# Whole-tile magnitudes taken in turn by ScalarE and VectorE, and the side work moved, in a long-convolution and MLP kernel

## The reference

```python
# part 1, per batch (2) over 12480 positions and 128 channels
h_filt = (np.maximum(pos_emb @ w1, 0.0) @ w2) * window
y = irfft(rfft(x * v, n=2*S) * rfft(h_filt, n=2*S))[:, :S]
x = (x * y).reshape(24960, 128)
# part 2
h = x @ w_in                      # 24960 x 2048
P = a[0] + a[1]*h + a[2]*h*h + a[3]*h*h*h
Q = 1.0 + abs(b[0])*abs(h) + abs(b[1])*h*h
out = (P / (Q + 1e-06)) @ w_out   # 24960 x 128
```

## Time and profile before

| what | value |
|---|---|
| median of 3 runs | 2174.0 us (2173.65 to 2177.25) |
| the profiled execution | 2174.0 us |
| its span in the trace | 2172.2 us |
| granted TensorE clock, mean | 0.983 |
| MLP stage, first slope to last slope | 630.1 to 2157.6 us |
| busy over the span | PE 92%, POOL 87%, DVE 84%, ACT 84% |

### The profile page before, as it was taken

One profiled execution on the slowest core, in us unless ns is written; L12 is line 12 of the kernel. 1 busy time (PEld: TensorE's weight loads), 2 busy tenths in 40 slices (PEclk: granted clock), 3 DMA queues, 4 the chain that ended last, 5 costly groups with the idle time before them and its releaser, 6 DMA issues. The chain is left out here.

```text
span 2172.2 us, 33906 instructions
## 1 busy us (share of the span) xinstructions
PE 2009.2 (92%) x8964; PEld 1463.6 (67%) x8964; DVE 1832.5 (84%) x2511; ACT 1824.1 (84%) x2671; POOL 1892.2 (87%) x1218
## 2 busy tenths in 40 slices
PE   7999499999959999999999999999999999999997
PEld 4777499999936666666666666666666666666664
DVE  4888488888849898989898988989888988898987
ACT  4888466666649998999999989999998989998998
POOL 3777398888839999999999999999999999999997
PEclk9999799999969999999999999999999999999999
DMA  6999766677531111111111111111111111111100
GB/s 178 312 305 309 191 162 172 178 181 180 128 86 31 31 31 31 30 31 30 31 30 31 34 31 31 30 33 50 36 31 31 30 31 30 31 30 31 30 13 12
DMA packets 65791, 175.60 MB, mean 81 GB/s; under 512 B 5046, under 2 KB 8414, under 8 KB 62686
## 3 DMA queue, kind: packets, MB, share of 16 engines
q1 hardware_dynamic: 65694, 174.67, 29.5%
HBM read 102.89 MB, written 71.76 MB: 80 GB/s over the span
## 5 line engine op out<-in xcount | busy, mean ns | idle before, releaser
L635 POOL TENSOR_TENSOR den<-slope,mag 128x832 f32<-128x832 f32 x480 | 948.1, 1975 | 43.4 <-POOL slope L627 4.6
L879 PE MATMUL acc_p<-g_s,w_out_k 128*128 128x416 f32 x1920 | 775.8, 527 | 61.3 <-DVE oT L801 38.5
L760 DVE SCALAR_TENSOR_TENSOR num<-square,level,h_p 128x832 f32<-128x832 f32 x480 | 517.7, 1078 | 116.2 <-ACT square L668 82.6
L627 POOL TENSOR_SCALAR slope<-mag,den_c 128x832 f32<-128x832 f32 x480 | 500.3, 1042 | 79.6 <-ACT mag L660 46.3
L879 PEld LDWEIGHTS acc_p<-g_s,w_out_k 128*128 128x128 f32 x1920 | 343.4, 190 | 315.5 <-issue 184.6
L793 DVE SCALAR_TENSOR_TENSOR g_s<-num,ratio,r_p 128x832 f32<-128x832 f32 x480 | 517.6, 1078 | 41.0 <-ACT r_p L684 26.8
L668 ACT ACTIVATE square<-h_p,centre 128x832 f32<-128x832 f32 x480 | 477.9, 996 | 7.7 <-DVE mag L755 5.3
L868 PE MATMUL h_p<-xy_hi,w_lo 128*128 128x416 f32 x960 | 448.5, 467 | 32.1 <-DVE num L760 29.5
L677 ACT ACTIVATE den<-den 128x832 f32<-128x832 f32 x480 | 450.1, 938 | 21.2 <-POOL den L635 21.1
L684 ACT ACTIVATE r_p<-den 128x832 f32<-128x832 f32 x480 | 436.2, 909 | 0.7 <-DVE g_s L793 0.7
L868 PE MATMUL h_p<-xy_lo,w_hi 128*128 128x416 f32 x960 | 338.0, 352 | 0.0
(11 more groups left out here) (79 smaller groups left out, 2807.9 us busy)
## 6 DMA issues: line engine op xcount, KB each, us to landing
bent<-bent_s SPq DMA_DIRECT2D x60, 576.0 KB, 6.2
bin_s<-bent SPq DMA_DIRECT2D x24, 1440.0 KB, 9.7
x_s<-in_x SPq DMA_DIRECT2D x60, 416.0 KB
back<-back_s SPq DMA_DIRECT2D x24, 960.0 KB, 7.8
vin_s<-back SPq DMA_DIRECT2D x30, 768.0 KB, 5.9
v_s<-in_v SPq DMA_DIRECT2D x30, 416.0 KB
out<-o_s SPq DMA_DIRECT2D x60, 208.0 KB
pos_s<-in_pos_emb SPq DMA_DIRECT2D x30, 88.0 KB
```

The costliest lines, as they stand in the source:

```text
L627: nc.gpsimd.tensor_scalar(slope[:, q % DEEP], mag[:, q % DEEP], den_c[:, 1:2], den_c[:, 0:1], ALU.mult, ALU.add).then_inc(slope_done, 1)
L635: nc.gpsimd.tensor_tensor(den[:, q % DEEP], slope[:, q % DEEP], mag[:, q % DEEP], ALU.mult).then_inc(den_done, 1)
L760: nc.vector.scalar_tensor_tensor(out=num[:, q % NUMS], in0=square[:, q % SQUARES], scalar=level[:], in1=h_p[:, q % 2, :, 0:TOK], op0=ALU.a ...
L879: mm = nc.tensor.matmul(acc_p[:, 0:TOK], w_out_k[:, ft], g_s[:, q % DEEP, t], start=(ft == 0), stop=(ft == FT - 1))
```

## The change

Four things are changed, all in the MLP stage:

- Whole tiles instead of halves: ACT takes the magnitude of even tiles (832 elements), DVE that of odd tiles. POOL waits for the one that made it. The square of an odd tile still waits for DVE's magnitude of this tile, the square of an even one no longer does.
- ACT's magnitude and square come right behind the reciprocal, ahead of leave and split_hi.
- DVE's sums stand at the head of a step, ahead of magnitude and activation; times_x and split_lo stand behind the numerator.
- PE's turn_in stands behind hidden and rows. The side work has other step numbers.

```diff
-            UNFOLD, TIMES_X, TURN_IN, SPLIT_HI, SPLIT_LO = (2, 5), (4, 7), (4, 7), (5, 8), (5, 8)
+            UNFOLD, TIMES_X, TURN_IN, SPLIT_HI, SPLIT_LO = (2, 6), (3, 7), (3, 7), (5, 9), (5, 9)
@@ pool, slopes
-                    pool.wait_ge(mag_act, G + 1)
-                    pool.wait_ge(mag_dve, G + 1)
+                    if q % 2:
+                        pool.wait_ge(mag_dve, i * (PER // 2) + q // 2 + 1)
+                    else:
+                        pool.wait_ge(mag_act, i * (PER // 2) + q // 2 + 1)
@@ act
-                    nc.scalar.activation(mag[:, q % DEEP, 0], h_p[:, q % 2, 0, 0:TOK], ACT.Abs).then_inc(mag_act, 1)
+                    nc.scalar.activation(mag[:, q % DEEP], h_p[:, q % 2, :, 0:TOK], ACT.Abs).then_inc(mag_act, 1)
 
                 def squared(i, q):
                     G = i * PER + q
                     act.wait_ge(h_done, G + 1)
-                    act.wait_ge(mag_dve, G + 1)
+                    if q % 2:
+                        act.wait_ge(mag_dve, i * (PER // 2) + q // 2 + 1)
...
                 def from_h(i, q):
-                    magnitude(i, q)
+                    if q % 2 == 0:
+                        magnitude(i, q)
                     squared(i, q)
@@ act, step
                     reciprocal(i, q)
+                    if ahead:
+                        from_h(i + (q + LEAD_E) // PER, (q + LEAD_E) % PER)
                     if m in LEAVE:
...
-                    if ahead:
-                        from_h(i + (q + LEAD_E) // PER, (q + LEAD_E) % PER)
@@ dve, magnitude
-                    nc.vector.tensor_scalar(mag[:, q % DEEP, 1].bitcast(I32), h_p[:, q % 2, 1, 0:TOK].bitcast(I32), NO_SIGN, None,
+                    nc.vector.tensor_scalar(mag[:, q % DEEP].bitcast(I32), h_p[:, q % 2, :, 0:TOK].bitcast(I32), NO_SIGN, None,
@@ dve, step
-                    if ahead:
-                        magnitude(i + (q + LEAD_E) // PER, (q + LEAD_E) % PER)
-                    activation(i, q)
                     if m in SUMS:
                         c = blk * BATCH + SUMS.index(m) - 1
                         if positive(c + 1):
                             sums(c)
-                    if more and m in TIMES_X:
-                        times_x(...)
-                    if more and m in SPLIT_LO:
-                        split_lo(...)
+                    if ahead and (q + LEAD_E) % 2:
+                        magnitude(i + (q + LEAD_E) // PER, (q + LEAD_E) % PER)
+                    activation(i, q)
                     if ahead:
                         numerator(i + (q + LEAD_E) // PER, (q + LEAD_E) % PER)
+                    side()          # times_x and split_lo, as above
@@ pe, step
                     project(i, q)
-                    if more and m in TURN_IN:
-                        turn_in(nxt + TURN_IN.index(m))
                     if ahead:
                         hidden(i + (q + LEAD_H) // PER, (q + LEAD_H) % PER)
                     if more and m in UNFOLD:
...
                         rows(nxt + half, i + (q // BLOCK_PAIRS + 1) // SLOTS, s, half, freed)
+                    if more and m in TURN_IN:
+                        turn_in(nxt + TURN_IN.index(m))
```

More of the change, by code:

```diff
@@ L808, in _ @@
                 for q in range(LEAD_E):
-                    magnitude(0, q)
+                    if q % 2:
+                        magnitude(0, q)
                     numerator(0, q)
@@ L813, in step @@
                     blk, m = i * SLOTS + q // BLOCK_PAIRS, q % BLOCK_PAIRS
-                    nxt, s = (blk + 1) * 2, (q // BLOCK_PAIRS + 1) % SLOTS
-                    if ahead:
-                        magnitude(i + (q + LEAD_E) // PER, (q + LEAD_E) % PER)
-                    activation(i, q)
                     if m in SUMS:
@@ L821, in step, with side @@
                             sums(c)
-                    if more and m in TIMES_X:
-                        times_x(nxt + TIMES_X.index(m), i + (q // BLOCK_PAIRS + 1) // SLOTS, s, TIMES_X.index(m))
-                    if more and m in SPLIT_LO:
-                        split_lo(nxt + SPLIT_LO.index(m), s, SPLIT_LO.index(m))
+                    if ahead and (q + LEAD_E) % 2:
+                        magnitude(i + (q + LEAD_E) // PER, (q + LEAD_E) % PER)
+                    activation(i, q)
+                    def side():
+                        nxt, s = (blk + 1) * 2, (q // BLOCK_PAIRS + 1) % SLOTS
+                        if more and m in TIMES_X:
+                            times_x(nxt + TIMES_X.index(m), i + (q // BLOCK_PAIRS + 1) // SLOTS, s, TIMES_X.index(m))
+                        if more and m in SPLIT_LO:
+                            split_lo(nxt + SPLIT_LO.index(m), s, SPLIT_LO.index(m))
                     if ahead:
                         numerator(i + (q + LEAD_E) // PER, (q + LEAD_E) % PER)
+                        side()
+                    else:
+                        side()
                 for q in range(PER):
```

## The result

The changed kernel takes 2199.1 us (median of 4 runs, 2197.7 to 2200.1), against 2174.5 for the kernel before on the same chip: ratio 1.011, 95% interval 1.0093 to 1.0128. It is slower, as forecast, but by 25 us and not by 94: only a quarter of the forecast loss came. The time lies 7 us above the low end of the range. The span of the profiled execution is 2195.5 us.

A forecast was written before the change was run, and what follows sets the result against it. A ring through ACT and DVE was to bound the MLP stage: 239.5 x 6.45 = 1544.8, + 23.8 splits + 22.4 loop gap + 30 sums = 1621.0 us against 1527.5. Forecast 2268 us, range 2192 to 2300.

The forecast's parts named there:

- The ring: MLP stage, ACT and DVE waiting in turn over an even and an odd tile: 6.45 us per two steps.
- split_hi: On ACT at steps 5 and 9, between odd square and logarithm: 0.41 us each, 58 times, 23.8 us.
- the sums at m = 8: On DVE ahead of activation, behind PE's late project: the numerator 1.0 us late, 30 times, 30 us.
- the leaves: On ACT at steps 2 and 14, behind the even square: 0.47 us each, hidden in a 0.75 us wait.
- DVE side work: times_x and split_lo behind an odd numerator on DVE, 0.6 us: hidden within 0.1 us.
- the wait for turn_in: ACT's wait for PE at split_hi: 1.53 x 4 = 6.1 us per 32 steps, forecast to go.
- Rival 1: MLP stage: POOL becomes the bound and the kernel gets faster, 2128 us; chance 0.08.
- rivals 2 and 3: MLP stage: 2, ring holds, split_hi and sums absorbed, 2214 us, chance 0.12; 3, ring low, extras absorbed, within 0.2%, 0.04.
- rival 4: PE's hidden matmuls of an odd tile come late behind rows, 60 times 0.4 us: about 2292 us; chance 0.10.
- The loop gap: On ACT where its loop jumps back, between odd square and logarithm: stays, 1.87 us x 12 = 22.4 us.
- The sums at m = 0: On DVE at the head of step 0: sums end at 6.3 us, the even numerator is not late, no cost.
- the low bound: Ring through ACT and DVE with shorter magnitudes and 0.09 us latency: 6.26 us; with sums free, 2192 us.

The follow-up runs named there:

- padded kernel: Changed kernel with two more, already met, waits per tile in ACT's program: 2221.6 us, ratio 1.0208 to the kernel before.
- the last experiment: Changed kernel with magnitudes in halves on both engines and DVE's sums behind the activation: 2158.4 us, ratio 0.9917 to the kernel before.

## Why the prediction was wrong in size

**The ring was right.** The odd square waits for DVE's magnitude behind the even numerator, the ring sets the pace, split_hi adds its 0.41 (0.40 measured), the sums at m = 8 their 1.0 (0.96), the leaves and the DVE side work nothing; the wait for turn_in goes. Undoing the sums gave 32 us (39 were expected), hiding the splits 22 us more (24 expected), a version with whole tiles alone shows the same 6.21, and with halves the plain pairs fall to 5.61. Rival 1 (POOL as the bound), rivals 2 and 3 (splits and sums absorbed) and rival 4 (PE's h late) are out: the pairs at 4 and 8 carry the extras, and between 800 and 2100 us neither ACT nor DVE waited for PE's h.

**Two terms were mis-sized, and one was wrongly put at nothing.** The forecast stage was 1621.0 us, measured 1548.4.

1. "Sum: 6.45 us for two steps." It is 6.21, and 239.5 x 0.24 = 57 us of the 73 are here. The piece from DVE's magnitude to the odd square was 1.05 and not 1.18: I took the half's 0.75 with the 0.17 behind its end as a fixed cost of that wait, but behind the whole magnitude the square starts within 0.03 (1506.14 + 1.02 = 1507.16, start 1507.19). The trace tells why the row misled: at the earlier trace rows the wait for the magnitude is held by an instruction of its own, with a register operation between it and the square, while in the changed kernel the square mostly holds the wait itself. The piece from ACT's whole magnitude to the even square was 0.74 and not 0.84: I scaled by the square, and the o_s copy, which gave 0.76, was the nearer row. Both low values were in the bounds, which with a shorter DVE magnitude gave 6.26; the ring lies just below even this. The errors look small, but a ring counts them 240 times.
2. "The loop gap: ... 1.87 x 12 = 22.4 us." It wasn't there. I carried the row over as a property of the jump, where it goes with the number of instructions in the body, and the change takes 19 of 281 out. The padded kernel, at 294, has the gap and is 22.5 us slower.
3. The sums at m = 0 went the other way: forecast free, measured 0.37 and 0.30, 10 us. The forecast had the even numerator due 7.45 us after the even square before it, and ready at 7.3. In one such place (square at 1464.76) it started 7.50 after it, because PE finished the batch 0.17 later than summed, and with the shorter ring it was due at 7.20.

Together: 57 + 22 - 10 + 2 for small terms = 71 of 73.

**The likeliest case and the range.** The range began at 2192 and held the measured 2199, but the forecast's own range (2235 to 2290) did not. The low value came from setting the sums to nothing and keeping the gap; the kernel had a ring just under the low bound, the sums, and no gap. That the range held the result is luck: what its low end left out and what it had too much nearly cancelled.

## What to carry to other kernels

Where two engines wait for each other in turn, add the starts round the ring before adding up the work of each engine: in the changed kernel the fullest engine, PE, was busy 189 of the 200 us from 1400 to 1600, and the ring decided. Each instruction on it counted in full, while the same instruction in a slot where its engine waits anyway was free. Making instructions fewer and longer saves time on their engine (DVE 1.02 us for a whole magnitude, 0.58 for each half) and lengthens the wait of whoever could go on with less. Here whole tiles made the kernel faster than before only once the side work was moved off the ring, and whether they beat halves in the same order was not shown. The stall at ACT's loop jump went with the number of instructions in the body, so a change to an engine's program can remove or bring it, whatever it does to the work. That number is read from the trace, not from the lines of the program.

## What was not expected of the hardware

- ACT's magnitude of 832 elements takes 0.74 us to the next start where the square of the same shape from the same buffer takes 0.84 to 0.86. The square also reads a bias tile; no run separates this.
- ACT's loop of 32 steps stalls at each jump back in the kernels with 278 to 294 instructions in the body (80 to 82 packets of instructions, a gap of 1.3 to 2.0 us) and not in those with 262 (20 or 21 packets, none); the limit lies between 262 and 278 here, as far as it is the length that decides.
- The delay from the end of DVE's magnitude to ACT's waiting square goes with the instruction of ACT that holds the wait. It is 0.03 to 0.04 us where the square holds it itself (143 waits of the changed kernel, 143 of the padded one), 0.08 where a wait instruction just ahead holds it (31 in the changed kernel; the last experiment), 0.11 where a register operation does (13), and 0.17 in the earlier trace rows, where a register operation stands between the wait and the square (13).
